# Batch 1's token transposes moved from TensorE to VectorE blocks and DMAs

## The reference

```python
def _moe2_ref(x, g_ln, w_ch1, w_ch2):
    mu = np.mean(x, axis=-1, keepdims=True)
    var = np.mean((x - mu) ** 2, axis=-1, keepdims=True)
    xn = (x - mu) / np.sqrt(var + 1e-06) * g_ln
    ch = np.maximum(xn @ w_ch1, 0.0) @ w_ch2
    return (x + ch).astype(np.float32)
```

## Time and profile before

| | |
|---|---|
| median of three runs | 469.66 us (469.55 to 470.8) |
| profiled execution, its own time | 470.99 us |
| its span in the trace | 469.3 us |
| TensorE matmul busy | 456.4 us, 97% of the span |
| VectorE busy | 278.2 us, 59% |
| ScalarE busy | 200.0 us, 43% |
| GpSimd busy | 269.6 us, 57% |
| TensorE's share of the chain that ended last | 87% |

### The profile page before, as it was taken

The page is one execution under the profiler, slowest core; times in us unless marked ns, Lnnn a source line. Parts: engine busy times, 40 slices in busy tenths (PEclk is TensorE's granted clock), DMA queues, the critical chain, the costliest instruction groups (busy, mean ns, idle before and its releaser), DMA issues.

```text
span 469.3 us, 8657 instructions
## 1 busy us (share of the span) xinstructions
PE 456.4 (97%) x3143; PEld 403.6 (86%) x3143; DVE 278.2 (59%) x625; ACT 200.0 (43%) x499; POOL 269.6 (57%) x409
## 2 busy tenths in 40 slices
PE   7899979999999999999999999999999999999997
PEld 6677658999998988989899888989998999899985
DVE  4879885787666877894655443466652334243333
ACT  2979968533334756445333342324310331233110
POOL 3645787999975000077988788780024488878100
PEclk9999999999999999999999999999999999999999
DMA  9988871121201100001122202210020202220003
GB/s 232 185 191 184 191 188 56 46 91 45 91 0 48 43 1 0 1 0 47 51 85 89 88 4 91 89 56 35 1 112 22 70 23 89 90 81 12 0 1 134
DMA packets 61702, 33.61 MB, mean 72 GB/s; under 512 B 44608, under 2 KB 55900, under 8 KB 61660
## 3 DMA queue, kind: packets, MB, share of 16 engines
q1 hardware_dynamic: 57788, 32.09, 24.2%
q10 hardware_dynamic: 3872, 0.97, 0.9%
HBM read 28.72 MB, written 3.15 MB: 68 GB/s over the span
## 4 chain that ended last, share of the span: by engine, by line
PE 87%; DVE 5%; SPq 2%; issue 2%; DMA 1%; ACT 1%; ACTq 1%; POOL 0%; DVEq 0%; POOLq 0%
PE two L1468 9%; PE two L1467 9%; PE two L1466 9%; PE two L1443 8%; PE two L1446 8%; PE two L1445 8%; PE two L1291 5%; PE two L1293 5%; PE two L1292 5%; PE two L1373 5%; PE two L1372 5%; PE two L1371 5%; DVE sm L649 2%; SPq L389 2%; PE two L1276 1%
## 5 line engine op out<-in xcount | busy, mean ns | idle before, releaser
L573 POOL TENSOR_TENSOR asum<-wst 128x256 f32<-128x256 f32 x26 | 23.2, 891 | 92.6 <-PE two L1293 50.2
L1443 PE MATMUL two<-combo,wa 128*128 128x384 f32 x224 | 75.7, 338 | 0.0
L1446 PE MATMUL two<-combo,wa 128*128 128x384 f32 x224 | 75.4, 337 | 0.0
L1468 PE MATMUL two<-wv,h 128*128 128x512 f32 x192 | 75.3, 392 | 0.0
L1467 PE MATMUL two<-wv,h 128*128 128x512 f32 x192 | 75.2, 392 | 0.0
L1445 PE MATMUL two<-combo,wa 128*128 128x384 f32 x224 | 75.2, 336 | 0.0
L1466 PE MATMUL two<-wv,h 128*128 128x512 f32 x192 | 75.0, 391 | 0.0
L536 POOL TENSOR_SCALAR pn<-ex,rinv 128x120 f32<-128x120 f32 x96 | 33.2, 365 | 24.7 <-DVE rinv L662 24.7
L567 POOL TENSOR_TENSOR wa<-asum,wa 128x256 fp32r<-128x256 f32 x52 | 43.5, 837 | 4.3
L602 POOL TENSOR_TENSOR wa<-wst,wa 128x256 fp32r<-128x256 f32 x39 | 29.6, 787 | 26.5 <-ACT wa L1069 26.5
L1291 PE MATMUL two<-xT,win 128*128 128x384 f32 x128 | 43.5, 340 | 0.0
(11 more groups left out here) (114 smaller groups left out, 985.2 us busy)
## 6 DMA issues: line engine op xcount, KB each, us to landing
wst<-in_moe_w_ch SPq DMA_DIRECT2D x26, 512.0 KB, 3.3
vW<-in_v SPq DMA_DIRECT2D x14, 240.0 KB
kn<-in_k SPq DMA_DIRECT2D x15, 192.0 KB, 3.7
qn<-in_q SPq DMA_DIRECT2D x15, 192.0 KB, 3.7
out<-y SPq DMA_DIRECT2D x11, 256.0 KB, 2.0
wst<-in_moe_w_in SPq DMA_DIRECT2D x8, 256.0 KB, 3.5
wst<-in_moe_w_out SPq DMA_DIRECT2D x8, 256.0 KB, 2.8
vW<-vs SPq DMA_DIRECT2D x16, 72.0 KB
```

Of the source, the lines that this page charges most:

```text
L1443: nc.tensor.matmul(o, wk[:, 0, kk], ck[:, 0, kk], start=(first and kk == 0), stop=False, skip_group_check=True)
L1446: ins = nc.tensor.matmul(o, wk[:, 1, kk], ck[:, 0, kk], start=False, stop=(kk == 1), skip_group_check=True)
L1468: ins = nc.tensor.matmul(o, lo, vh, start=False, stop=(f == NFP - 1 and c == 1), skip_group_check=True)
```

## The change

For batch 1 `tokens_t` is no longer called. VectorE transposes each centred tile in blocks of 32x32 into a new tile `xq` (`turn_blocks`), right after its centring. `xq` has room for three tiles, so the turn of tile 3 writes where tile 0's lay and waits until the first move has ended. In a block transpose the 32 values of a block change partitions among themselves only, so block (a, d) of a 128x128 square still has to go from partitions 32a to partitions 32d. SyncE does that with 16 DMAs for each three tiles (`move_tokens`), straight into `tok`; ScalarE then scales `tok` in place, four slots in unit 4 and four in unit 5.

```diff
-        TOK_UNIT = {2: {1: 0, 2: 1}, 3: {1: 2, 2: 3}, 4: {1: 4, 2: 5}, 5: {1: 6, 2: 7}}
+        TOK_UNIT = {4: range(4), 5: range(4, 8)}
...
-        tok = at("tok", [P, 4, 2, HALF], F32, XT_AT)
+        tok = at("tok", [P, 2, KD, HALF], F32, XT_AT)
...
+        xq = at("xq", [P, KD, 3, P], F32, HG_AT + 2 * 2 * S * 4)
+        xn1 = [at("xn1_0", [P, DM], F32, XT_AT + XT_B + SLOT_B),
+               at("xn1_1", [P, DM], F32, WIO_AT + 5 * COMBO_B)]
...
+            def move_tokens(t):
+                sp.wait_ge(xq_done, 3 * (t + 1))
+                if t == 0:
+                    sp.wait_ge(combo_done, NPROD)
+                for a in range(4):
+                    for d in range(4):
+                        src = xq[32 * a:32 * (a + 1)].rearrange("p k i (d c) -> p (k i) d c", c=32)[:, :, d]
+                        dst = tok[32 * d:32 * (d + 1), t].rearrange("p k (i a c) -> p (k i) a c", a=4, c=32)[:, :, a]
+                        sp.dma_start(dst, src).then_inc(tok_in, 16)
...
                 load_a(l)
                 load_v2(l)
+                if l in (5, 6):
+                    move_tokens(l - 5)
...
                     dve.wait_ge(tile_proj, T * 2 * KF)
-                    if i == 3:
-                        dve.wait_ge(xt_ready, NSLOT + KD)
+                    if i >= 2:
+                        dve.wait_ge(xq_done, i - 1)
...
+            def turn_blocks(i):
+                dve.wait_ge(xn_done, T + i + 1)
+                if i == 3:
+                    dve.wait_ge(tok_in, 16 * 16)
+                nc.vector.transpose(xq[:, :, i % 3], xn_home(1, i).rearrange("p (k d) -> p k d", k=KD)).then_inc(xq_done, 1)
...
                     for i in range(3):
                         centre(1, i)
+                        turn_blocks(i)
...
                     for i in range(3, T):
                         centre(1, i)
+                        turn_blocks(i)
...
-                act.wait_ge(xt_ready, NSLOT * b + slot + 1)
-                if b >= 1:
-                    act.wait_ge(combo_done, NPROD * b)
-                nc.scalar.activation(tok[:, 2 * (k // 2) + t, k % 2], src[:, 0:HALF], ACT.Copy,
-                                     scale=cols[:, k:k + 1]).then_inc(xr_done, 1)
+                if b == 0:
+                    act.wait_ge(xt_ready, slot + 1)
+                else:
+                    act.wait_ge(tok_in, 16 * 16 * (t + 1))
+                nc.scalar.activation(tok[:, t, k], src, ACT.Copy, scale=cols[:, k:k + 1]).then_inc(xr_done, 1)
...
-                for i in sorted(slots):
-                    tokens(1, slots[i], a)
+                for slot in slots:
+                    tokens(1, slot, tok[:, slot // KD, slot % KD])
...
-                if i in TOK_UNIT.get(g, {}):
-                    pe.wait_ge(h2_done, 4 * g + 1)
-                    tokens_t(1, TOK_UNIT[g][i], ps_h[g % 2])
...
-                if g in TOK_UNIT:
-                    pe.wait_ge(xr_done, NSLOT + TOK_UNIT[g][2] + 1)
                 product(g, 4)
```

More of the change, by code:

```diff
@@ L209, in conv_gated_attention_kernel @@
         xn_done, xt_ready, xr_done = sem("xn_done"), sem("xt_ready"), sem("xr_done")
+        xq_done, tok_in = sem("xq_done"), sem("tok_in")
         tsum_done, ch_done, combo_done = sem("tsum_done"), sem("ch_done"), sem("combo_done")
@@ L319, in xn_home, with token_block @@
         def xn_home(b, i):
-            return xn0[:, i] if b == 0 else xn1[i][:]
+            return xn0[:, i] if b == 0 else xn1[i % 2][:]
+        def token_block(kh, t):
+            return tok[:, t, 2 * kh:2 * kh + 2]
         A_PLACE = (0, 2, 5, 4, 1, 6, 3)
         def combo_src(k):
-            return (tok[:, 0], tsum[:, 0], tok[:, 2], tsum[:, 1], tok[:, 1], tsum[:, 2], tok[:, 3])[k]
+            return (token_block(0, 0), tsum[:, 0], token_block(1, 0), tsum[:, 1], token_block(0, 1), tsum[:, 2],
+                    token_block(1, 1))[k]
         def h2_block(g, k):
@@ L350, in token_sum @@
         def token_sum(i):
-            b11, b12, b21, b22 = tok[:, 0], tok[:, 1], tok[:, 2], tok[:, 3]
+            b11, b12, b21, b22 = token_block(0, 0), token_block(0, 1), token_block(1, 0), token_block(1, 1)
             t2, t3, t4 = tsum[:, 0], tsum[:, 1], tsum[:, 2]
@@ L1109, in _ @@
                         if i in at_tile:
-                            tokens(0, at_tile[i], ps_h[at_tile[i] % 2])
+                            tokens(0, at_tile[i], ps_h[at_tile[i] % 2][:, 0:HALF])
                     sigmoid(s)
                 if 4 in at_tile:
-                    tokens(0, at_tile[4], ps_h[at_tile[4] % 2])
+                    tokens(0, at_tile[4], ps_h[at_tile[4] % 2][:, 0:HALF])
                 if s == KF:
@@ L1131, in _ @@
                 a = ps_h[g % 2]
-                slots = TOK_UNIT.get(g, {})
+                slots = TOK_UNIT.get(g, ())
                 act.wait_ge(prod_done, NPROD * g + 1)
@@ L1375, in project, with tokens_t @@
                     ins.then_inc(tile_proj, 1)
-            def tokens_t(b, slot, dst):
+            def tokens_t(slot, dst):
                 t, k = slot // KD, slot % KD
[L1381 to L1384, removed]
+                pe.wait_ge(xn_done, 3 * t + 3)
+                if slot >= 2:
                     pe.wait_ge(xr_done, slot - 1)
                 for i in range(3):
-                    ins = nc.tensor.transpose(dst[:, P * i:P * (i + 1)], xn_home(b, 3 * t + i)[:, P * k:P * (k + 1)],
+                    ins = nc.tensor.transpose(dst[:, P * i:P * (i + 1)], xn_home(0, 3 * t + i)[:, P * k:P * (k + 1)],
                                               ident[:])
@@ L1412, in _ @@
                         pe.wait_ge(h_done, 2 * (s + 1))
-                        tokens_t(0, TOK_TILE[s][i], ps_h[TOK_TILE[s][i] % 2])
+                        tokens_t(TOK_TILE[s][i], ps_h[TOK_TILE[s][i] % 2])
             project(2 * KF - 2, range(T))
```

## The result

The changed kernel takes 483.57 us (median of 4, 481.75 to 484.86) against 470.12 (median of 4, 469.55 to 470.8): ratio 1.0281, 95% interval 1.0244 to 1.0317. It is 13.4 us slower. The profiled execution took 484.86 us, its span 483.1.

What follows compares the result with a forecast made beforehand. TensorE's issue was taken to bound the kernel. Terms -2.8 + 0.15 + 11.2 + 1.5 = +10.1 us on the median of 469.66 gave 479.8 us, range 475 to 488.

Steps and rivals of the forecast that it cites:

- transposes and their waits gone: TensorE, units 2 to 5: 24 transposes and the waits around them go, 0.70 us a unit, -2.8 us.
- `u2` late in unit 2: VectorE, unit 2: three block transposes of 0.66 us ahead of `u2` cost 0.15 us with the release.
- first DMA goes out at: SyncE: the first move waits behind `load_v2(5)`, issued at 265.3, so its first DMA goes out at 265.7.
- move, D: Length of one move of 16 DMAs: 15 x 0.50 plus 2.3 for landing, 9.8 us; bounds 7.9 to 16.0.
- from the move to `c21` done: VectorE, unit 3: three turns, two centrings, `c21` and their waits after the move, 3.8 us, done at 279.3.
- TensorE stands: Before product 0 of unit 4, TensorE waits for `c21` of unit 3 from 268.1 to 279.3, 11.2 us.
- lower clock behind it: First three products of unit 4 at 1.2 GHz after the gap: 0 to 3.1 us, middle 1.5 taken.
- dear pieces: Rival, chance 0.20: DMA engines set the move, 128-byte pieces cost twice 14.3 ns; D 13.3, +14.9, 484.5 us.
- the second move stays hidden: Unit 5: ScalarE waits for move 1 until +6.3, `h2_high` 0.5 us late; hidden from TensorE below D of 12.
- Dear turns: Rival, chance 0.05: VectorE's block transposes take 1.51 us each, 2.7 us more in units 2 and 3 each; 485.2.
- A light move: Rival, chance 0.06: low end of D and no loss of clock, +6.6, 476.3 us; perhaps 473 to 475.
- The move is covered: Rival, chance 0.04: `tok_in` is full before VectorE reaches the turn in unit 3; only -2.8 remains, 467 us.

Runs made afterwards that it cites:

- the early start: Against the changed kernel, the first move stands in SyncE's queue behind load 4 instead of load 5; 468.21 us, ratio 0.9957 to the kernel before.
- the two runs with work in the gap: Changed kernel plus useless small matmuls on TensorE before product 0 of unit 4: 112 with a pause, 484.75 us; 100 without, 484.91 us.

## Why the prediction was right

Counted from `c21` of unit 1, so without the 1.30 us from the attention layer:

| step | forecast, us | measured, us | from |
|---|---|---|---|
| transposes and their waits gone | -2.8 | -2.7 | run without them |
| `u2` late in unit 2 | +0.15 | +0.2 | `c21` of unit 2: 252.99 - 1.30, against 252.21 - 0.70 |
| first DMA goes out at | 265.7 | 265.5 | 266.82 - 1.30 |
| move, D | 9.8 | 12.1 | 278.93 - 266.82 |
| from the move to `c21` done | 3.8 | 3.5 | 281.91 + 0.52 - 278.93 |
| TensorE stands | +11.2 | +13.2 | 282.58 - 269.24 - 0.17 |
| lower clock behind it | +1.5 | +2.0 | 5.13 - 3.14 |
| sum | +10.1 | +12.7 | 12.5 between the traces |

The median came out at 483.57 us against the 479.8 forecast: inside the range of 475 to 488, but above the forecast's own band of 475.5 to 482.5, and nearer to the rival of the dear pieces (484.5). 0.5 us of the difference is the median before, which is 470.12 with the fourth execution and was 469.66 in the forecast.

The mechanism was right in each step: what holds the move back, who waits for it in which order, where TensorE stops, and that the second move stays hidden (ScalarE waited 4.96 us in unit 5 and `c21` there still waited 0.85 us for TensorE). Only the bound for that was too strict: from 12 us upwards each further microsecond of a move was to stop TensorE, and the second move took 13.1 (295.86 to 308.97) and stopped nothing. The start of the move was forecast within 0.2 us, from the 1.88 us that ScalarE's casts no longer cost.

The term that was mis-sized is D, at 12.1 us against 9.8, still inside the bounds of 7.9 to 16.0. The step was "I take 0.50, the row with that form and 16 engines". That row loads from HBM; with the source in HBM the same DMAs take 0.47 to issue, and the move then 9.7 us, by the run that put it there. With both ends in SBUF it is 0.62, and 0.66 from one to the next. The only SBUF-to-SBUF row of before, 0.81, told of this, but the prediction used it for the high bound alone. The landing, 2.0 us, was near the 2.3 assumed. So 15 x 0.16 = 2.4 us of issue make up the error of D. The turns and centrings behind it gave 0.3 us back, and the clock added 0.5.

The rivals. *Dear pieces* had nearly the right time for a wrong reason: half the pieces changed nothing, and during the move the DMA engines' share was 0.47. The Trainium skill ("DMA: Bandwidth & Descriptors", Why small descriptors are slow (HBM only)) has it that transfers inside SBUF do not suffer from small descriptors. No run here tests that, since all the pieces have 128 bytes; half as many of them landed in 1.9 us instead of 2.0. *Dear turns*: 0.71 us each, their starts 0.64 before the next instruction's, so near the low bound; unit 2 lost 0.2 us. *A light move* did not come: the landing of 2.0 us was near its low bound of 1.7, the 0.66 from one issue to the next was far from 0.41. *The move is covered* is what the early start makes of it, and then the change wins 1.7 us.

The clock: the price taken was the middle between nothing and 3.1 us, and 2.0 was measured; no row stood behind that middle, so its nearness is luck. The Trainium skill's rule of the idle array ("TensorE: Matmul & The Clock Gate", Part 1: The HAM clock gate) agrees with the trace: the granted clock was 0.50 for the last 8 us of the gap and came back between 286 and 288 us, while the products ran. In the two runs with work in the gap the clock fell too, though TensorE had stood for only 0.58 and 2.33 us before; why, no run here shows.

## What to carry to other kernels

A transfer that replaces work on the busiest engine costs what its first waiting reader costs, so look at two places before its bytes: what stands ahead of it in the queue that issues it, and what stands behind the instruction that waits for it. Giving the waiting instruction its own buffer only handed the wait to the next reader here; starting the transfer when its data was ready removed it, with one line. Where many small DMAs are needed, count them and multiply by an issue from a row with the same two ends, since neither bytes nor pieces set the time here.

## What the runs showed of the hardware that I had not expected

- What one issue costs SyncE, by kind: 0.33 us for a store to HBM, 0.37 for a load of 512 KB, 0.47 for 32 partitions with 12 pieces of 128 bytes from HBM, 0.62 for the same from SBUF to SBUF, 0.81 for another kind from SBUF to SBUF. Only the 0.47 and the 0.62 differ in nothing but the source. Half the pieces (0.61) or four times the partitions (0.63) made little difference.
- Small matmuls of 128 columns, 0.113 us each, held TensorE's granted clock at 1.0 for 11.3 us; then it fell during the kernel's own matmuls, behind a gap of 2.33 us. In the attention layer the trace before shows no fall behind a wait of 1.83 us, and the trace after shows one at a wait of 1.10, so in these rows the length of the wait alone does not tell.
- A VectorE transposition of 128x512 float32 in blocks takes 0.71 us, and the next instruction starts 0.64 after it.
